# One-hot rows of a token router compared in bf16, with two tokens innermost

## The reference, cut to what matters

```
y = irfft(rfft(x, axis=1) * (filt_r + 1j * filt_i), n=3072, axis=1)       # float32
x = y.reshape(24576, 256)
expert_idx = argmax(x @ w_gate);  gate_w = softmax(x @ w_gate)[expert_idx]
for i in range(N):                       # in order
    e = expert_idx[i]
    if counts[e] < capacity:
        disp[e, counts[e]] = x[i];  pos[i] = counts[e];  counts[e] += 1;  keep[i] = True
h = relu(disp @ w1);  y = h @ w2         # per expert, 256 -> 1024 -> 256
out[i] = gate_w[i] * y[expert_idx[i], pos[i]]   if keep[i], else 0
```

## Time and profile before

| | us |
|---|---|
| median of 3 runs | 497.0 (496.35 to 500.02) |
| the profiled execution: its own time | 496.46 |
| the profiled execution: span of the trace | 494.6 |
| PE busy | 453.8 (92%) |
| DVE busy | 243.0 (49%) |
| ACT busy | 215.4 (44%) |
| POOL busy | 188.8 (38%) |

### The profile page before, as it was taken

The page is one execution under the profiler, slowest core; times in us unless marked ns, Lnnn a source line. Parts: engine busy times, 40 slices in busy tenths (PEclk is TensorE's granted clock), DMA queues, the critical chain, the costliest instruction groups (busy, mean ns, idle before and its releaser), DMA issues.

```text
span 494.6 us, 12093 instructions
## 1 busy us (share of the span) xinstructions
PE 453.8 (92%) x5160; PEld 399.2 (81%) x5160; DVE 243.0 (49%) x380; ACT 215.4 (44%) x402; POOL 188.8 (38%) x159
## 2 busy tenths in 40 slices
PE   5989999896998878989979999999999999999993
PEld 5855558555774464979969999999999999999993
DVE  1095526899499965791453242363134344224300
ACT  2745555351455546621544253455434345423310
POOL 0000000000000050386467887566786457584122
PEclk9999999998999999999999999999999999999998
DMA  8994989859943354822132794411795310970011
GB/s 301 404 401 137 345 260 323 290 205 329 320 136 120 136 209 129 279 87 86 43 118 66 239 404 167 138 45 33 242 403 184 129 43 27 345 268 23 33 35 36
DMA packets 45743, 93.02 MB, mean 188 GB/s; under 512 B 5840, under 2 KB 20848, under 8 KB 45168
## 3 DMA queue, kind: packets, MB, share of 16 engines
q1 hardware_dynamic: 39408, 79.50, 45.8%
q0 software_dynamic: 6272, 12.65, 7.7%
HBM read 46.49 MB, written 45.64 MB: 186 GB/s over the span
## 4 chain that ended last, share of the span: by engine, by line
PE 79%; DVE 12%; issue 4%; DMA 2%; ACT 1%; POOLq 0%; POOL 0%; SPq 0%; DVEq 0%; ACTq 0%
PE psum L1269 27%; PE psum L1255 25%; DVE prod L787 5%; PE psum L489 4%; PE psum L506 4%; PE psum L473 4%; PE psum L546 3%; PE psum L503 3%; PE psum L642 2%; PE psum L580 2%; PE psum L536 2%; PE psum L522 1%; DVE hot_lo L912 1%; DVE prod L795 1%; PE psum L576 1%
## 5 line engine op out<-in xcount | busy, mean ns | idle before, releaser
L1083 DVE SCALAR_TENSOR_TENSOR hl<-psum,hh 128x384 fp32r<-128x384 f32 x128 | 69.6, 556 | 144.4 <-ACT hh L1034 144.4
L1269 PE MATMUL psum<-w2h,hh 128*128 128x256 f32 x384 | 109.9, 286 | 0.0
L1269 PE MATMUL psum<-w2h,hl 128*128 128x256 f32 x384 | 108.8, 283 | 0.0
L1269 PE MATMUL psum<-w2l,hh 128*128 128x256 f32 x384 | 108.8, 283 | 0.0
L1034 ACT ACTIVATE hh<-psum 128x384 fp32r<-128x384 f32 x128 | 62.1, 492 | 61.5 <-PE psum L1255 61.3
L1255 PE MATMUL psum<-xh,w1h 128*128 128x384 f32 x256 | 86.2, 337 | 2.1 <-DVE hl L1083 2.0
L1255 PE MATMUL psum<-xh,w1l 128*128 128x384 f32 x256 | 85.7, 335 | 0.0
L1255 PE MATMUL psum<-xl,w1h 128*128 128x384 f32 x256 | 85.7, 335 | 0.0
L787 DVE TENSOR_TENSOR prod<-psum,fab 128x1024 f32<-128x1024 f32 x48 | 56.5, 1218 | 47.2 <-PE psum L473 38.9
L1171 POOL DMA_INDIRECT out<-o_out,token x48 | 50.2, 1047 | 70.5 <-ACT o_out L1043 56.7
L1269 PEld LDWEIGHTS psum<-w2l,hh 128*128 128x128 f32 x384 | 73.7, 192 | 0.0
(11 more groups left out here) (109 smaller groups left out, 540.7 us busy)
## 6 DMA issues: line engine op xcount, KB each, us to landing
out<-zero SPq DMA_DIRECT2D x24, 1024.0 KB, 12.3
w_raw<-in_w SPq DMA_DIRECT2D x14, 1024.0 KB, 5.8
x_in<-in_x SPq DMA_DIRECT2D x18, 512.0 KB, 6.4
t_scratch<-t_out SPq DMA_DIRECT2D x24, 256.0 KB, 4.1
z_in<-t_scratch SPq DMA_DIRECT2D x32, 192.0 KB, 3.9
y_rows<-y SPq DMA_DIRECT2D x12, 512.0 KB, 2.8
fab<-in_fab SPq DMA_DIRECT2D x4, 1024.0 KB, 14.4
first_raw<-in_w SPq DMA_DIRECT2D x2, 1024.0 KB, 8.2
```

The costliest lines, as they stand in the source:

```text
L1083: nc.vector.scalar_tensor_tensor(out=hl[:, b % 2, f, :], in0=ps[(2, 3, 6, 7)[f % 4]][:, 0:TOK], scalar=0.0, in1=hh[:, b % 2, f, :].bitcast ...
L1269: mm = nc.tensor.matmul(ps[4 + (b * ST + s) % 2][:, 0:D], hx[:, b % 2, f, s * P:(s + 1) * P], wt[k][:, f, :], start=(f == 0 and m == 0), s ...
```

## The change

`lo`, `hi` (new tile `digits`), the numbers 0 to 128 (new tile `pairs`, each number twice in a row) and the digits of the tokens' numbers (new tile `tokens16`) are now bf16. The one-hot arrays are laid out with the tokens in pairs: `[token pair, number, 2]` in place of `[token, number]`, so that the innermost two elements of every operand belong to two neighbouring tokens. The weights and the moving operand of the table's matmuls are now picked out of these pairs with a step of two elements. Two copies, which make `pairs` and `tokens16`, are added on DVE behind the sums of the last step of part 0, with a wait there for the constants. `zero` moves to another place in the list of tiles.

```diff
+        pairs = sb("pairs", [P, P + 1, 2], BF16)
+        tokens16 = sb("tokens16", [P, 4, N2], BF16)
+        tok_hi, tok_lo, half_hi, half_lo = (tokens16[:, i, :] for i in range(4))
+        digits = sb("digits", [P, 2, N2], BF16)
...
-        hot_lo = sb("hot_lo", [P, N2, P], BF16)
-        hot_eq = sb("hot_eq", [P, N2, NHI], BF16)
-        hot_hi = sb("hot_hi", [P, N2, 2, NHI], BF16)
+        hot_lo = sb("hot_lo", [P, HN, P, 2], BF16)
+        hot_eq = sb("hot_eq", [P, HN, NHI, 2], BF16)
+        hot_hi = sb("hot_hi", [P, 2, HN, NHI, 2], BF16)
...
+        def by_pair(a):
+            return a.rearrange("p (n two) -> p n two", two=2)
...
-                mm = nc.tensor.matmul(table_in(into), hot_lo[:, n, :],
-                                      hot_hi[:, n].rearrange("p k h -> p (k h)"), start=(n == 0), stop=(n == N2 - 1))
+                mm = nc.tensor.matmul(table_in(into), hot_lo[:, n // 2, :, n % 2], hot_hi[:, :, n // 2, :, n % 2], start=(n == 0), stop=(n == N2 - 1))
...
+                if t == 0 and h == NG - 1:
+                    dve.wait_ge(consts, 16 * 4)
+                    nc.vector.tensor_copy(pairs[:, :, :], nums[:, 0:P + 1].unsqueeze(2).to_broadcast(
+                        [P, P + 1, 2])).then_inc(spread_set, 1)
+                    nc.vector.tensor_copy(tokens16[:, :, :].rearrange("p k n -> p (k n)"), of_tokens).then_inc(spread_set, 1)
...
-                ins = nc.vector.tensor_scalar(hi, hi, -ROUND, None, ALU.add)
+                ins = nc.vector.tensor_scalar(hi16, hi, -ROUND, None, ALU.add)
...
-                k = slice((n - ONE_HOT) * N2 // 3, (n - ONE_HOT + 1) * N2 // 3)
-                ins = nc.vector.tensor_tensor(hot_lo[:, k, :], lo[:, k].unsqueeze(2).to_broadcast([P, N2 // 3, P]),
-                                              lo_numbers.unsqueeze(1).to_broadcast([P, N2 // 3, P]), ALU.is_equal)
+                if t == 0 and n == ONE_HOT:
+                    dve.wait_ge(spread_set, 2)
+                k = slice((n - ONE_HOT) * HN // 3, (n - ONE_HOT + 1) * HN // 3)
+                ins = nc.vector.tensor_tensor(hot_lo[:, k], by_pair(lo16)[:, k].unsqueeze(2).to_broadcast([P, HN // 3, P, 2]),
+                                              pairs[:, 1:P + 1, :].unsqueeze(1).to_broadcast([P, HN // 3, P, 2]), ALU.is_equal)
...
-                ins = nc.vector.tensor_tensor(hot_hi[:, :, 0, :], hot_eq[:, :, :],
-                                              (half_hi if t == HALF else tok_hi).unsqueeze(2).to_broadcast([P, N2, NHI]), ALU.mult)
+                ins = nc.vector.tensor_tensor(hot_hi[:, 0], hot_eq[:, :, :, :], by_pair(half_hi if t == HALF else tok_hi).unsqueeze(
+                    2).to_broadcast([P, HN, NHI, 2]), ALU.mult)
```

More of the change, by code:

```diff
@@ L232, in build @@
         y = sb("y", [P, 3, CH, D])
-        zero = sb("zero", [P, 512])
         lg_t = sb("lg_t", [P, NCH, P])
@@ L240, in build @@
         rows = sb("rows", [P, 3, E * N2])
[L241 to L245, removed]
+        zero = sb("zero", [P, 512])
+        nums = sb("nums", [P, P + 1 + 32 + 4 * N2])
+        pick, of_tokens = nums[:, P + 1:P + 33], nums[:, P + 33:]
+        pairs = sb("pairs", [P, P + 1, 2], BF16)
+        tokens16 = sb("tokens16", [P, 4, N2], BF16)
+        tok_hi, tok_lo, half_hi, half_lo = (tokens16[:, i, :] for i in range(4))
+        digits = sb("digits", [P, 2, N2], BF16)
         wgs = sb("wgs", [P, DH, 32])
@@ L289, in build @@
         wa_loaded, sq_loaded, consts, set_up, gaps_set = map(sem, ("wa_loaded", "sq_loaded", "consts", "set_up", "gaps_set"))
+        spread_set = sem("spread_set")
         x_loaded = [sem(f"x_loaded{i}") for i in range(NCH)]
@@ L840, in dve_route @@
             of_expert, resets, first_slot = (rows[:, k, :] for k in range(3))
-            top, index, total, norm, slot_, hi, lo = (small[:, k, :] for k in range(7))
+            top, index, total, norm, slot_, hi = (small[:, k, :] for k in range(6))
+            hi16, lo16 = (digits[:, k, :] for k in range(2))
             at = rank_at if ranked == 7 else 0
@@ L914, in dve_route @@
             elif n == ONE_HOT + 3:
-                ins = nc.vector.tensor_tensor(hot_eq[:, :, :], hi.unsqueeze(2).to_broadcast([P, N2, NHI]),
-                                              hi_numbers.unsqueeze(1).to_broadcast([P, N2, NHI]), ALU.is_equal)
+                ins = nc.vector.tensor_tensor(hot_eq[:, :, :, :], by_pair(hi16).unsqueeze(2).to_broadcast([P, HN, NHI, 2]),
+                                              pairs[:, 0:NHI, :].unsqueeze(1).to_broadcast([P, HN, NHI, 2]), ALU.is_equal)
@@ L917, in dve_route @@
             elif n == ONE_HOT + 4:
-                ins = nc.vector.tensor_tensor(hot_hi[:, :, 0, :], hot_eq[:, :, :],
-                                              (half_hi if t == HALF else tok_hi).unsqueeze(2).to_broadcast([P, N2, NHI]), ALU.mult)
+                ins = nc.vector.tensor_tensor(hot_hi[:, 0], hot_eq[:, :, :, :], by_pair(half_hi if t == HALF else tok_hi).unsqueeze(
+                    2).to_broadcast([P, HN, NHI, 2]), ALU.mult)
             elif n == ONE_HOT + 5:
-                ins = nc.vector.tensor_tensor(hot_hi[:, :, 1, :], hot_eq[:, :, :],
-                                              (half_lo if t == HALF else tok_lo).unsqueeze(2).to_broadcast([P, N2, NHI]), ALU.mult)
+                ins = nc.vector.tensor_tensor(hot_hi[:, 1], hot_eq[:, :, :, :], by_pair(half_lo if t == HALF else tok_lo).unsqueeze(
+                    2).to_broadcast([P, HN, NHI, 2]), ALU.mult)
@@ L1459 @@
     earlier = (row[:, None] < row).astype(_np.float32)
-    numbers = _np.concatenate([_np.tile(_np.arange(1, P + 1), (P, 1)), _np.tile(_np.arange(NHI), (P, 1)),
-                               token // P + 1, token % P,
+    numbers = _np.concatenate([_np.tile(_np.arange(P + 1), (P, 1)),
                                _np.where(i[:, None] % 32 < E, i[:, None] // 32 * E + i[:, None] % 32 == _np.arange(32), 0),
-                               early // P + 1, early % P],
-                              1).astype(_np.float32)
+                               token // P + 1, token % P, early // P + 1, early % P], 1).astype(_np.float32)
     both = _np.stack([fr[order], fi[order]]).reshape(2, 2, QR, NG, NQ, D)
```

2 lines of the change are left out of this document (1 added, 1 removed).

## The result

| | before | changed |
|---|---|---|
| median us (4 runs each) | 496.7 | 491.8 (490.96 to 492.3) |
| ratio, 95% interval | | 0.988 (0.985 to 0.992) |
| the profiled execution: own time, span | 496.46, 494.6 | 491.62, 489.8 |
| DVE busy, PE busy | 243.0, 453.8 | 233.4, 455.6 |

A forecast was written before the change was run, and what follows sets the result against it. It took DVE to bound 109.51 to 124.37 us and part 2 from 136.05, PE most of the rest. Terms 1.8 + 3.4 + 1.9 = 7.1 us gave 490.0 us; likeliest 488.5 to 491.5, up to 494.5 with rivals.

The forecast's parts named there:

- the prediction's own sign of being wrong: Wrong as a whole if DVE saves its 10 us and part 2's L489 does not come 5.2 us earlier.
- price of a comparison: DVE at 0.517 ns an element: `hot_lo` 0.69 us (0.54 less), `hot_eq` and `hot_hi` 0.75 us (0.60 less).
- The dear end of the range: Upper bound for a DVE comparison with 16-bit operands: 1.042 ns an element as now, no gain.
- Part 2, -3.4: Routing of part 1: all six comparisons lie in the stretch that DVE bounds, so 3.4 us are gained.
- The narrow place that the walk found: Part 2, last L473: PE would start it at 166.9 and end at 168.0; DVE, at 168.1, is later by 0.1.
- Experts, -1.9: Routing of part 2: 0.54 us from PE's wait for `hl`, 1.34 from its wait before the third table.
- The two copies, 0: New DVE copies before the multiply at 74.45: at most 0.7 us, covered by 5.71 us of DVE idle time.
- Strided weights, 0: The table's 24 matmuls per part stay at 49 ns each with weights 4 bytes apart; up to 3.9 us otherwise.
- Part 1, -1.8: Routing of part 0: `hot_eq` and two `hot_hi` after 109.51, where DVE is alone, count in full, 1.8 us.
- PE must follow: Part 1 after 109.51: PE's steps are short (1.1 + 1.55 us against DVE's 3.65), so DVE's gain arrives.
- the prediction had a fall here cost nothing: Part 1, clock's fall at 118.3 to 122.3: PE's L489 and table end about 122.5, just when the sums end.
- rival D: Gain partly given back by a wait that nothing shows now; 493.4 us if half of 7.1 goes; 6%.

The follow-up runs named there:

- flat_bf16: The changed kernel with all operands still bf16 but the old layout, one token per row; ratio 0.999 (0.995 to 1.003) to the kernel before.
- zeros_spread: The changed kernel with four 1 MB stores of zeros issued one by one in part 2; 490.32 us, ratio 0.983 to the kernel before.
- zeros_later_after: The changed kernel with four 1 MB stores of zeros moved behind part 2's last loads; 493.62 us, ratio 0.989 to the kernel before.

## Why the prediction was right, and where its size was off

- **As a whole**: the time lay in the range, but the prediction's own sign of being wrong came up. DVE saved its 10 us (243.0 to 233.4), and the inverse transform at the end of part 2, L491, started at 172.20 in place of 175.25: 3.05 us earlier and not 5.2. What was right are the price of a comparison and two of the three terms; that the time came so near is in part luck, since single falls of the clock, which come with either kernel, cost 1.4 us and more, as much as was missing.
- **The price of a comparison**: right to 0.01 us. The dear end of the range, one element per 1.04 ns with 16 bits, is what the old layout gives (`flat_bf16`, 1.22 us); the reason given for the layout, two neighbours side by side in all three operands, held: with the pairs `hot_lo` takes 0.69. The price of L918, which I put down to its one wide operand, comes with the old layout even where all operands are bf16 (L929 in `flat_bf16`, 1.36 us), so no run shows what one wide operand costs by itself.
- **Part 2, -3.4**: right, 39.20 to 35.82 = 3.38, in all six traces where nothing else held PE up. The narrow place that the walk found was real: PE's L475 of step 7 starts at 167.14 with no wait, as forecast (166.9), and DVE is still the later:

```profile
167.14 1.09 PE L475 MATMUL psum<-z_in,wf 64*32 64x256 f32 x32
168.48 2.35 DVE L791 TENSOR_TENSOR prod<-psum,fab 128x1024 f32<-128x1024 f32 x2
```

- **Experts, -1.9**: right. By the chain, the first L1267 to the table takes 217.82 - 193.55 = 24.27 us against 222.90 - 196.75 = 26.15. The assumption that `hot_lo` is still held up by POOL's instruction stood: it took 3.05 us and ended 0.55 us behind POOL's instruction of 4.61 us (209.67):

```profile
205.06 4.61 POOL L1017 TENSOR_TENSOR w2l<-w_raw,w2h 128x2048 fp32r<-128x2048 f32 x1 [1.83 <-ACT w2h L1009]
207.17 3.05 DVE L924 TENSOR_TENSOR hot_lo<-digits,pairs 128x1024 bf16<-128x1024 bf16 x1
```

In all 14 traces this `hot_lo` starts inside POOL's instruction and takes 3.00 to 3.59 us; it ends 0.55 to 0.56 us behind it in the seven where part 2 is routed in bf16 pairs, and 1.08 to 1.09 in the seven others. What holds it is not shown.
- **The two copies, 0**: right, 0.41 and 0.20 us in front of a multiply before which DVE is still idle for 5.26. **Strided weights, 0**: right.
- **Part 1, -1.8**: the term that was mis-sized. DVE's stretch shrank by 1.81 us, or 1.51 in the changed kernel's first trace: there the clock was at its lower level (0.50 from 117.2 to 120.4 us) during the forward transform at 117.25, which took 1.96 us in place of 1.10 and held DVE up (the prediction had a fall here cost nothing). But PE then waits for instructions. Step 5 to the logits takes 18.4 us in the mean of the six traces with part 0 in float32 and the stores in place (17.8 to 18.75) and 17.7 in the three with part 0 in bf16 (17.0 to 18.3): 0.7 of 1.8 arrived. This is rival D, a load that shows no wait now on DMA engines that are full: I named it, at 6%, for the loads of part 2, and it was the fetch of instructions, which had left its mark in the page: PE idle with the releaser "issue" in the middle of a group, 1.62 us that end at 91.65 and 0.22 at 127.15. I read these as nothing. The step that failed is "PE must follow": PE's steps are short enough, but its instructions are not there.
- **The sum.** From 494.6 to 489.8 by the two traces: part 1's sums -1.5, the break +1.7, part 2 -3.4, from part 2's end to the table -2.0, the lower clock behind the gather and what goes with it +1.2, the start +0.2, and what lies behind the last matmuls -0.9, which differs by as much between two traces of one kernel: -4.7, and -4.8 is measured. The change itself is worth 7.1 - 1.1 = 6.0 us by the traces, or 0.988; the ratio measured is the same, but its interval would also hold 4.0 or 7.5 us.

## What to carry to other kernels

Halving the width of both operands of these comparisons paid only when the innermost two elements of every operand lay side by side, also of the one that is broadcast (0.69 us for `hot_lo`, against 1.22): put two independent items innermost. Before counting a gain on a path that goes back to PE, look for "issue" waits in the middle of a group of matmuls: here PE was held there to the time at which its instructions arrived, and DVE's gain did not move that time (the packet started at 124.87 before and at 124.79 with the change). Four stores of 1 MB in a row, with the DMA share at 1.03, delayed the instructions; the same stores one at a time, where the engines had room (`zeros_spread`, DMA share 0.70 from 130 to 170 us), cost nothing.

## What the runs showed of the hardware

- A 16 KB packet of PE's instructions came late enough to stop PE for 0.2 to 3.3 us beside busy DMA engines (share 1.03 from 117 to 126.3 us before the 1.88 in the changed kernel, 1.01 from 148 to 165 us before the 3.33 in `zeros_later_after`, but 0.87 from 86.5 to 90 us before the 1.06 that ends at 91.83 in the changed kernel). That the late thing is this packet is shown by the places (60 of 60 breaks) and by the packets, whose end each break follows by 1.20 to 1.76 us. That the stores cause the breaks in question is shown by moving them and leaving them out. It need not be stores: the breaks at 34, 39 and 77 us fall before the first store of zeros is issued (81 us), beside loads and `t_scratch` (DMA share 1.03 from 30 to 34 us, 0.74 from 35.5 to 38.5 us and 1.03 from 73 to 78 us in the changed kernel).
- POOL's indirect DMAs were shorter beside the fast comparisons. Beside the old ones (215.3 to 222.8) two took 1.74 and 1.73 us; in the changed kernel, beside `hot_eq`, 0.99. It is not the width: in `flat_bf16`, bf16 at one element per 1.04 ns, they took 1.74 and 1.72. Why is not shown. POOL's timeline, before and then changed:

```profile
215.67 1.74 POOL L1155 DMA_INDIRECT o_gate<-gate_rows,token  x1 [0.31 <-issue]
217.72 1.73 POOL L1155 DMA_INDIRECT o_gate<-gate_rows,token  x1 [0.30 <-issue]
```

```profile
213.76 0.99 POOL L1167 DMA_INDIRECT o_gate<-gate_rows,token  x1 [0.30 <-issue]
```

- The lower clock (0.50, for 3.4 or 6.8 us at a time in these traces) came after idle stretches of PE, but not after each: behind the gather, where PE idled 2.45 to 2.56 us in every trace, in 6 of 14. At the end of part 2 it came in 4 of the 6 traces where PE idled 2.1 to 2.2 us before the last inverse transform, and in none of the 8 where it idled less. A fall there cost 1.3 us (`flat_bf16`, 0.50 for 3.4 us) or 2.7 us (the other three, 6.8 us). The change shortens this idle stretch from 2.19 to 1.32 us, so it may gain on average what none of the terms has; the traces are too few to show it.
